# An mLSTM followed by two dense layers: the order of the TensorE program from block 1 on, two steps at a time

## The chip, the cores and the metric

The kernel runs on one core of a Trainium2 chip (trn2). The metric is the device time of one execution in microseconds (us); lower is better. Before the change the median of three runs was 830.93 us (830.81 to 833.44).

## What is computed

```python
# attention: batch 4, heads 8, sequence 768, head size 40, all float32
for t in range(S):
    m_new = np.maximum(f_gate[:, :, t] + m, i_gate[:, :, t])
    f_stab = np.exp(f_gate[:, :, t] + m - m_new)
    i_stab = np.exp(i_gate[:, :, t] - m_new)
    C = f_stab * C + i_stab * outer(v_t, k_t)
    n = f_stab * n + i_stab * k_t
    y[:, :, t] = sigmoid(o_gate_t) * (C @ q_t) / max(abs(n . q_t), 1)
x = y as [3072 tokens, 320]
# first dense layer (320 -> 2048 -> 320)
h = x @ w_in;  g = relu(h) ** 2;                x = g @ w_out
# second dense layer, its own weights
h = x @ w_in2; g = where(h > 0, h, exp(h) - 1); x = g @ w_out2
```

## The kernel before, in words

**Tiles, blocks and steps.** The 3072 tokens are 24 tiles of 128 (tile g is chunk g // 4 of batch g % 4). Three tiles (384 tokens) are a block, 8 blocks make a dense layer, and the two layers are blocks 0 to 7 and 8 to 15. The hidden size 2048 is cut into 16 slices of 128 (`NF`). A **step** is one slice of one block: step t is slice j = t % 16 of block t // 16, 256 steps in all.

**The two products of a step.** TensorE makes the hidden values of a step with `first_product(t)` (line 990, matmuls on line 1000), called F(j) here: 8 matmuls of 128x384 into one of two PSUM banks, `hps[t % 2]`. Values are split in a high and a low part, of which the products that matter are summed. `second_product(t)` (line 1004, matmuls on line 1014), called S(j), adds the step's part to the three accumulators of the block: 9 matmuls of 128x320 into `acc`. S runs `LAG = 3` steps behind F. F(j) waits until the values of step j - 2 have been read from its bank (`relu_ready` in layer one, `g_ready` in layer two); S waits for `glo_ready` of its step.

**Between F and S, layer one.** ScalarE takes relu (line 576), squares it into the high part `ghi` (579) and into `gfull` (580); VectorE subtracts the two to get the low part `glo` (825). ScalarE's relu of step t waits for `glo` of step t - 2, since `relu` and `gfull` have two buffers.

**Between F and S, layer two.** VectorE takes the minimum with zero (857), ScalarE the exponential (618), VectorE the combination (862, `g_ready`), ScalarE the high part (623), GpSimd the low part (456).

**The attention** of tiles 3 to 23 is spread over the steps of blocks 0 to 6 of layer one. `start_of(g)` gives the step s in which a tile starts; `tile_at(t, delay)` finds the tile with s + delay = t. From block 1 on the three tiles of a block start at slices 15 (of the block before), 4 and 9; they are called A, B and C here. On TensorE: `scores` in step s (line 889), `state_added` and `from_state` in step s + 2 (905, 916), `within` in step s + 3 (925). On VectorE: `weigh` in s (659), `gate_recip` in s + 2 (648), `update_state`, `add_inter` and, behind `glo`, `finish` in s + 3 (690 to 707), the transposes of the tile's result in s + 4 (`turned`, 721, 16 instructions), `x_lo` in s + 5 (712), which makes the input of the next block ready (`xt_ready`), and `split_k_lo` of the next tile in its step s - 2 (644). On ScalarE: `exponents` (494), `split_k_hi` in s - 3 (468), `split_q_hi` in s - 2 (473), `x_hi` in s + 5 (509), which waits for the transposes. On GpSimd: `mask` (372) in s - 3, `make_wv` (384) in s - 2, `split_q_lo` in s - 1 (367, two instructions).

**Layer two** has no attention. VectorE transposes the next block's input (721) in the 12 slices of `X2_TURNS`, two instructions behind the minimum and two behind the combination, and makes its low part (`x2_lo`, 733) in slices 5 and 10 behind the combination and in slice 15 ahead of the minimum. It waits each time for `x2_hi` (504) on ScalarE.

**What sets the order.** Each engine runs its own list in program order, written out by hand; semaphores tie them together. TensorE's list before is F(j), the attention of step j, S(j - 3), for each j; at j = 0 the second product comes first and there is none behind. So F(0) and F(1) of a block already stand side by side, and so do the second products of slices 12 and 13. ScalarE's `empty_acc` (526) copies the finished accumulators of a block out in step 2 of the next.

Of the kernel before, what the change touches and what calls it, by code (L numbers as in the profile page):

```python
# [20 lines left out]
NF = FF // P  # L21
T = 3
NT = T * P
BLOCKS = TILES // T
# [36 lines left out]
def tile_at(t, delay):  # L61

    for g in range(T, TILES):
        if start_of(g) + delay == t:
            return g
    return None
# [13 lines left out]
def mlstm_two_dense_layers(nc, gates_ends, gates_inner, qk, q_trios, kvo, w_all, m_dram, out):  # L80
    with ExitStack() as ctx:
# [382 lines left out]
        def _(act):  # L464
# [61 lines left out]
            def empty_acc(block):  # L526
                for u in range(T):
                    i = T * block + u
                    act.wait_ge(s["g_used"], T * (NF * (block + 1) - 1) + u + 1)
                    if block < BLOCKS:  # L530
                        nc.scalar.activation(x2[:, i, :], acc[u][:, 0:DM], ACT.Copy).then_inc(s["acc_free"], 1)
                    else:
                        wait_stage = 16 * (block - BLOCKS)
                        if wait_stage:
                            act.wait_ge(out_done[u], wait_stage)
                        nc.scalar.activation(out_stage[u], acc[u][:, 0:DM], ACT.Copy).then_inc(s["acc_free"], 1)
# [33 lines left out]
            for block in range(2 * BLOCKS):  # L570
                for j in range(NF):
                    t = NF * block + j
                    if block < BLOCKS:
                        act.wait_ge(s["h_ps"], t + 1)
                        wait(act, "glo_ready", t - 1)
                        nc.scalar.activation(relu[t % 2], hps[t % 2][:, 0:NT], ACT.Relu).then_inc(s["relu_ready"], 1)  # L576
                        act.wait_ge(s["relu_ready"], t + 1)
                        wait(act, "g_used", T * (t - GR + 1))
                        nc.scalar.activation(ghi[t % GR][:], relu[t % 2], ACT.Square).then_inc(s["ghi_ready"], 1)  # L579
                        nc.scalar.activation(gfull[t % 2], relu[t % 2], ACT.Square).then_inc(s["g_ready"], 1)  # L580
                        if t + EARLY < NF:
                            split_hi(t + EARLY)
                            split_out_hi(t + EARLY)
                        if FROM_ACT <= t + RING + EARLY - BEHIND < NF:
                            load_w(act, t + RING + EARLY - BEHIND)
                        g = tile_at(t, -5)
                        if g is not None and g >= B:
                            exponents(g, 0)
                        g = tile_at(t, -4)
                        if g is not None and g >= B:  # L590
                            exponents(g, 1)
                        g = tile_at(t, -3)
                        if g is not None and g >= B:
                            split_k_hi(g)
                        g = tile_at(t, -2)
                        if g is not None and g >= B:
                            split_q_hi(g)
                        g = tile_at(t, -1)
                        if g is not None and g >= B:
                            out_gate(g)  # L600
                        if t in FIRST_STATES:
                            first_state(FIRST_STATES[t])
                        g = transposed_at(t)
                        if g is not None:
                            x_hi(g, (g // T) % 2, g % T, A2 if g < 2 * T else x1_turned)
                        if j == LAG - 1 and block > 0:
                            empty_acc(block - 1)
                        if block == BLOCKS - 1:
                            if j >= 1:
                                split_hi(NF + j - 1)  # L610
                            if j >= LAG + 1:
                                split_out_hi(NF + j - LAG - 1)
                            if j in X2_STEPS:
                                w = X2_STEPS.index(j)
                                x_hi(TILES + w, 0, w, (A0, A1, A2)[w])
                    else:
                        act.wait_ge(s["hneg_ready"], t - NF * BLOCKS + 1)
                        nc.scalar.activation(relu[t % 2], relu[t % 2], ACT.Exp).then_inc(s["e_ready"], 1)  # L618
                        if j == LAG - 1:
                            empty_acc(block - 1)  # L620
                        act.wait_ge(s["g_ready"], t + 1)
                        act.wait_ge(s["g_used"], T * (t - GR + 1))
                        nc.scalar.activation(ghi[t % GR][:], gfull[t % 2], ACT.Copy).then_inc(s["ghi_ready"], 1)  # L623
                        if block == BLOCKS and j < LAG + 1:
                            if j == 0:
                                split_hi(2 * NF - 1)
                            split_out_hi(2 * NF - LAG - 1 + j)
                        if block < 2 * BLOCKS - 1 and j in X2_HI_STEPS:
                            w = X2_HI_STEPS.index(j)
                            x2_hi(T * (block + 1 - BLOCKS) + w, (block + 1) % 2, w)  # L630
# [242 lines left out]
        def _(pe):  # L873
            def scores(g):
                if g < B:
                    pe.wait_ge(s[f"qk_in_{g}"], 16)
                    q_h, k_h = q_raw(g), k_raw(g)
                else:
                    pe.wait_ge(s["k_lo"], with_state(g) + 1)
                    q_h, k_h = q3, k3  # L880
                if g >= T:
                    pe.wait_ge(s["den_ready"], g)
                if g == T:
                    pe.wait_ge(s["decay_ready"], 1)
                for u, bank in enumerate(score_banks(g)):
                    if g >= B:
                        pe.wait_ge(s["q_lo"], 2 * with_state(g) + u + 1)
                    for h in range(HH):
                        last = nc.tensor.matmul(bank[:, h * P:(h + 1) * P], k_h[:, u * HH + h, :], q_h[:, u * HH + h, :],  # L889
                                                start=True, stop=True)  # L890
                    last.then_inc(s["s_ps"], 1)

            def state_added(g):
                if chunk_of(g) == CH - 1:
                    return
                pe.wait_ge(s["wv_ready"], g + 1)
                if g == 0:
                    pe.wait_ge(s["a_col_ready"], 2)
                elif g <= T:
                    pe.wait_ge(s["state_ready"], g)  # L900
                else:
                    pe.wait_ge(s["xt_ready"], min(g, 2 * T))
                    pe.wait_ge(s["state_ready"], g)
                for h in range(H):
                    last = nc.tensor.matmul(A2[0:D, h * E:(h + 1) * E], k_of(g)[:, h, :], wv[:, h, :], start=True, stop=True)  # L905
                last.then_inc(s["dc_ps"], 1)
# [111 lines left out]
                if j < NF - 1:  # L1018
                    last.then_inc(s["g_used"], T)

            for block in range(2 * BLOCKS):
                for j in range(NF):
                    t = NF * block + j
                    if j == 0 and block > 0:
                        second_product(t - LAG)
                    first_product(t)
                    if t in FIRST_STATES:
                        state_added(FIRST_STATES[t])
                    g = tile_at(t, 0)
                    if g is not None:  # L1030
                        scores(g)
                    g = tile_at(t, 2)
                    if g is not None:
                        if g > T:
                            state_added(g)
                        from_state(g)
                    g = tile_at(t, 3)
                    if g is not None:
                        within(g)
                    if block == BLOCKS - 1 and j in X2_STEPS:  # L1040
                        w = X2_STEPS.index(j)
                        x2_transposed(w, w)
                    if t >= LAG and j > 0:
                        second_product(t - LAG)
                    g = transposed_at(t)
                    if g is not None and g < 2 * T:
                        x1_transposed(g)
            for t in range(2 * BLOCKS * NF - LAG, 2 * BLOCKS * NF):
                second_product(t)

# [44 lines left out]
```

## Time and profile before

| | |
|---|---|
| median of three runs | 830.93 us |
| the profiled execution, its own time | 832.15 us |
| its span | 830.3 us |
| TensorE matmul busy | 824.3 us, 99% |
| TensorE weight load busy | 813.5 us, 98% |
| VectorE busy | 634.7 us, 76% |
| ScalarE busy | 492.8 us, 59% |
| GpSimd busy | 260.6 us, 31% |
| share of the chain that ended last, by engine | PE 96%, DVE 2%, DMA 1%, ACT 1% |

The span is the time from the first to the last instruction of the program; the execution's own time holds the launch around it. PE is TensorE's matmuls, PEld its weight loads, DVE VectorE, ACT ScalarE, POOL GpSimd, SP SyncE. L1000 is line 1000 of the kernel. The chain that ended last is followed back from the last instruction, at each step to what released it.

### The profile page before, as it was taken

What the parts mean: (1) busy time and instruction counts of PE and PEld (TensorE: products, weight loads), DVE (VectorE), ACT (ScalarE), POOL (GpSimd) and SP (SyncE); (2) the same over time, 40 slices, a digit from 0 to 9 for tenths busy, and PEclk for the clock granted to TensorE, in tenths of its full rate; (3) what the DMA queues carried; (4) which work ended last, traced back from release to release, by engine and by line L of the source; (5) the groups of instructions that cost most, each with busy time, mean ns of one, the idle gap of its engine ahead of it and who ended that gap; (6) DMA issues with size and microseconds to landing.
All of it is one profiled execution on the core that took longest, in us unless ns stands there. A gap on an engine that the chain in (4) does not pass through costs nothing.

```text
span 830.3 us, 15300 instructions
## 1 busy us (share of the span) xinstructions
PE 824.3 (99%) x5451; PEld 813.5 (98%) x5451; DVE 634.7 (76%) x1447; ACT 492.8 (59%) x1088; POOL 260.6 (31%) x270
## 2 busy tenths in 40 slices
PE   9999999999999999999999999999999999999998
PEld 7899999999999999999999999999999999999998
DVE  5798798888897988987966687777868777777642
ACT  4698675776766867678657754444444444444433
POOL 2664222322222222212102353333333333333332
DMA  7785444353653444445132300000000000000000
GB/s 250 241 229 149 136 119 110 109 132 90 160 150 80 140 119 110 109 110 147 46 105 70 106 3 4 27 4 26 2 28 3 28 3 27 4 26 5 2 24 25
DMA packets 29939, 67.64 MB, mean 81 GB/s; under 512 B 9736, under 2 KB 17064, under 8 KB 27304
## 3 DMA queue, kind: packets, MB, share of 16 engines
q1 hardware_dynamic: 29288, 65.23, 27.8%
q10 hardware_dynamic: 576, 1.44, 0.5%
q8 instruction: 43, 0.70, 0.3%
q14 instruction: 32, 0.26, 0.1%
HBM read 60.87 MB, written 4.03 MB: 78 GB/s over the span
## 4 chain that ended last, share of the span: by engine, by line
PE 96%; DVE 2%; DMA 1%; ACT 1%; issue 0%; POOL 0%; DVEq 0%
PE hps L1000 44%; PE acc L1014 41%; PE att L925 5%; PE att L889 2%; PE att L916 2%; PE att L905 2%; DMA wts<-m_rows 1%; ACT wts L494 1%; DVE gate L648 0%; DMA m_rows<-x 0%; DVE wts L659 0%; DMA x<-in_gates_ends 0%; PE att L930 0%; DVE x L704 0%; DVE xtl L712 0%
## 5 line engine op out<-in xcount | busy, mean ns | idle before, releaser
L1000 PE MATMUL hps<-xth,win 128*128 128x384 f32 x1280 | 351.4, 340 | 0.0
L1014 PE MATMUL acc<-wout,ghi 128*128 128x320 f32 x1536 | 345.0, 311 | 0.0
L1000 PE MATMUL hps<-xtl,win 128*128 128x384 f32 x768 | 260.2, 339 | 0.0
L1014 PEld LDWEIGHTS acc<-wout,ghi 128*128 128x128 f32 x1536 | 259.4, 188 | 0.0
L1014 PE MATMUL acc<-wout,glo 128*128 128x320 f32 x768 | 237.4, 309 | 0.0
L1000 PEld LDWEIGHTS hps<-xth,win 128*128 128x128 f32 x1280 | 230.1, 189 | 0.3
L456 POOL TENSOR_TENSOR glo<-hact,ghi 128x384 fp32r<-128x384 f32 x128 | 130.2, 1018 | 215.4 <-ACT ghi L623 215.4
L1000 PEld LDWEIGHTS hps<-xtl,win 128*128 128x128 f32 x768 | 145.0, 189 | 0.0
L1014 PEld LDWEIGHTS acc<-wout,glo 128*128 128x128 f32 x768 | 144.0, 188 | 0.0
L618 ACT ACTIVATE hact<-hact 128x384 f32<-128x384 f32 x128 | 67.4, 526 | 122.3 <-DVE hact L857 122.3
L825 DVE TENSOR_TENSOR glo<-hact,ghi 128x384 fp32r<-128x384 f32 x128 | 75.9, 593 | 66.0 <-ACT hact L580 65.1
L623 ACT ACTIVATE ghi<-hact 128x384 fp32r<-128x384 f32 x128 | 67.3, 526 | 74.6 <-DVE hact L862 74.6
L576 ACT ACTIVATE hact<-hps 128x384 f32<-128x384 f32 x128 | 61.9, 483 | 82.5 <-PE hps L1000 82.5
L857 DVE TENSOR_SCALAR hact<-hps 128x384 f32<-128x384 f32 x128 | 71.1, 556 | 41.7 <-PE hps L1000 39.9
L862 DVE SCALAR_TENSOR_TENSOR hact<-hact,hps 128x384 f32<-128x384 f32 x128 | 71.0, 554 | 28.1 <-ACT hact L618 26.1
L721 DVE STREAM_TRANSPOSE x<-x 32x96 f32<-32x96 f32 (+1 forms) x336 | 84.9, 253 | 7.4
L372 POOL TENSOR_SCALAR_AFFINE_SELECT wts<-wts 128x1024 f32<-128x1024 f32 x24 | 26.3, 1096 | 188.8 <-ACT wts L494 188.6
L721 DVE STREAM_TRANSPOSE x_turned<-x 32x96 f32<-32x96 f32 x288 | 77.6, 269 | 3.6
L367 POOL TENSOR_TENSOR q<-raw,q 40x512 fp32r<-40x512 f32 x40 | 51.9, 1316 | 79.9 <-ACT q L473 79.7
L579 ACT ACTIVATE ghi<-hact 128x384 fp32r<-128x384 f32 x128 | 67.2, 525 | 4.0
L580 ACT ACTIVATE hact<-hact 128x384 f32<-128x384 f32 x128 | 65.0, 508 | 0.0
L494 ACT ACTIVATE wts<-wts,a_col 128x128 f32<-128x128 f32 x192 | 60.4, 387 | 2.1 <-DMA wts<-m_rows 2.1
(142 smaller groups left out, 729.7 us busy)
## 6 DMA issues: line engine op xcount, KB each, us to landing
raw<-in_qk SPq DMA_DIRECT2D x20, 960.0 KB, 7.1
wts<-m_rows SPq DMA_DIRECT2D x24, 512.0 KB, 8.5
kvo<-in_kvo SPq DMA_DIRECT2D x21, 484.0 KB, 7.9
x<-in_w_all SPq DMA_DIRECT2D x12, 352.0 KB, 5.5
wts<-in_w_all SPq DMA_DIRECT2D x12, 352.0 KB, 3.0
q_of_three<-in_q_trios SPq DMA_DIRECT2D x20, 180.0 KB, 2.7
out_x<-hsum SPq DMA_DIRECT2D x16, 160.0 KB, 1.9
x<-in_w_all ACTq DMA_DIRECT2D x4, 352.0 KB, 5.8
```

The source lines that it names most:

```text
L456: nc.gpsimd.tensor_tensor(glo[t % GR][:], gfull[t % 2], f32(ghi[t % GR][:]), ALU.subtract)\
L494: nc.scalar.activation(w[:, h, :], w[:, h, :], ACT.Exp, bias=a_col[:, c, r:r + 1], scale=-1.0).then_inc(s["exp_ready"], 1)
L579: nc.scalar.activation(ghi[t % GR][:], relu[t % 2], ACT.Square).then_inc(s["ghi_ready"], 1)
L580: nc.scalar.activation(gfull[t % 2], relu[t % 2], ACT.Square).then_inc(s["g_ready"], 1)
L618: nc.scalar.activation(relu[t % 2], relu[t % 2], ACT.Exp).then_inc(s["e_ready"], 1)
L623: nc.scalar.activation(ghi[t % GR][:], gfull[t % 2], ACT.Copy).then_inc(s["ghi_ready"], 1)
L721: last = nc.vector.transpose(blocks[q * 32:(q + 1) * 32, 0:n], rows[:, q::4])
L825: nc.vector.tensor_tensor(glo[t % GR][:], gfull[t % 2], f32(ghi[t % GR][:]), ALU.subtract)\
L857: nc.vector.tensor_scalar(relu[t % 2], hps[t % 2][:, 0:NT], 0.0, None, ALU.min).then_inc(s["hneg_ready"], 1)
L862: nc.vector.scalar_tensor_tensor(out=gfull[t % 2], in0=relu[t % 2], scalar=-1.0, in1=hps[t % 2][:, 0:NT], op0=ALU.add, op1=ALU.max).then_i ...
L1000: last = nc.tensor.matmul(hps[t % 2][:, 0:NT], win[:, j, w, :], x[:, kk, :], start=(i == 0), stop=(i == len(parts) - 1))
L1014: last = nc.tensor.matmul(acc[u][:, 0:DM], g[t % GR][:, cols], wout[:, j, w, :], start=(j == 0 and i == 0), stop=(j == NF - 1 and i == 2))
```

## The change

TensorE's program is reordered from block 1 on, and ScalarE's `empty_acc` is put one step earlier to go with it. No instruction is added or taken away. The attention part of a step becomes a function, with its calls in the order that they had. Block 0 keeps its order. From block 1 on TensorE takes slices j and j + 1 together: F(j), F(j + 1), the attention of both, then two second products. With the second product that stands first at j = 0, the list of a block is

S(13) F0 F1 S(14) S(15) | F2 F3 S0 | F4 F5 S1 S2 | F6 F7 S3 S4 | F8 F9 S5 S6 | F10 F11 S7 S8 | F12 F13 S9 S10 | F14 F15 S11 S12

where S(13) to S(15) are of the block before, and the attention of each pair stands behind its two F.

```diff
-                        if j == LAG - 1 and block > 0:
+                        if j == LAG - 2 and block > 0:
                             empty_acc(block - 1)
...
-                        if j == LAG - 1:
-                            empty_acc(block - 1)
                         act.wait_ge(s["g_ready"], t + 1)
                         act.wait_ge(s["g_used"], T * (t - GR + 1))
                         nc.scalar.activation(ghi[t % GR][:], gfull[t % 2], ACT.Copy).then_inc(s["ghi_ready"], 1)
+                        if j == LAG - 2:
+                            empty_acc(block - 1)
...
+            def attention(t):
+                block, j = divmod(t, NF)
+                if t in FIRST_STATES:
+                    state_added(FIRST_STATES[t])
+                g = tile_at(t, 0)
+                if g is not None:
+                    scores(g)
+                g = tile_at(t, 2)
+                if g is not None:
+                    if g > T:
+                        state_added(g)
+                    from_state(g)
+                g = tile_at(t, 3)
+                if g is not None:
+                    within(g)
+                if block == BLOCKS - 1 and j in X2_STEPS:
+                    w = X2_STEPS.index(j)
+                    x2_transposed(w, w)
+
+            for t in range(NF):
+                first_product(t)
+                attention(t)
+                if t >= LAG:
+                    second_product(t - LAG)
+                g = transposed_at(t)
+                if g is not None:
+                    x1_transposed(g)
+            for block in range(1, 2 * BLOCKS):
+                for j in range(0, NF, 2):
                     t = NF * block + j
-                    if j == 0 and block > 0:
+                    if j == 0:
                         second_product(t - LAG)
                     first_product(t)
...
-                    if t >= LAG and j > 0:
-                        second_product(t - LAG)
...
+                    first_product(t + 1)
+                    attention(t)
+                    attention(t + 1)
+                    if j != 2:
+                        second_product(t - LAG + (j == 0))
+                    second_product(t - LAG + 1 + (j == 0))
```

## Rows read from the trace of the kernel before

**Rows 1.** The page's line of busy time, share of the span and instructions by engine.

```profile
PE 824.3 (99%) x5451; PEld 813.5 (98%) x5451; DVE 634.7 (76%) x1447; ACT 492.8 (59%) x1088; POOL 260.6 (31%) x270
```

**Rows 2.** Waits of TensorE: who for whom, us in total, times, longest.

```profile
PE att L889 <- issue: 0.5, 2, 0.3
```

**Rows 3.** Timeline, TensorE, layer two: start us, us, engine, line, operation, tiles, count.

```profile
588.91 0.51 PE L1000 MATMUL hps<-xth,win 128*128 128x384 f32 x2
...
590.32 0.45 PE L1014 MATMUL acc<-wout,ghi 128*128 128x320 f32 x2
...
591.63 0.51 PE L1000 MATMUL hps<-xth,win 128*128 128x384 f32 x2
...
603.96 0.45 PE L1014 MATMUL acc<-wout,ghi 128*128 128x320 f32 x2
...
606.59 0.51 PE L1000 MATMUL hps<-xth,win 128*128 128x384 f32 x2
...
609.39 0.45 PE L1014 MATMUL acc<-wout,ghi 128*128 128x320 f32 x2
```

**Rows 4.** Timeline, VectorE and ScalarE, slices 10, 11 and 12 of a layer-two block.

```profile
590.52 0.56 DVE L857 TENSOR_SCALAR hact<-hps 128x384 f32<-128x384 f32 x1 [0.50 <-PE hps L1000]
...
593.23 1.06 DVE L733 TENSOR_TENSOR xtl<-x,xth 128x384 fp32r<-128x384 f32 x1 [1.01 <-ACT xth L504]
...
598.70 0.56 DVE L857 TENSOR_SCALAR hact<-hps 128x384 f32<-128x384 f32 x1
...
600.44 0.49 DVE L721 STREAM_TRANSPOSE x<-x 32x64 f32<-32x64 f32 x2
```

**Rows 5.** Timeline, VectorE and TensorE: a wait for `den_ready` (L704) ends at scores.

```profile
92.17 0.49 DVE L704 TENSOR_TENSOR x<-att,rden 128x320 f32<-128x320 f32 x1
...
92.76 0.41 PE L889 MATMUL att<-q,k 120*128 120x128 f32 x2 [0.25 <-issue]
```

**Rows 6.** Timeline, TensorE, end of a layer-one block: within, S9, and F0 of the next.

```profile
252.86 1.87 PE L925 MATMUL att<-kvo,wts 128*128 128x41 f32 x16
254.56 0.53 PE L1014 MATMUL acc<-wout,ghi 128*128 128x320 f32 x2
...
266.37 0.51 PE L1000 MATMUL hps<-xth,win 128*128 128x384 f32 x2
```

**Rows 7.** Timeline, VectorE, the same stretch: tile C from finish to x_lo.

```profile
255.03 0.50 DVE L690 TENSOR_TENSOR att<-hsum,att 128x328 f32<-128x328 f32 x1
...
256.99 0.20 DVE L707 COPY x<-x 128x64 f32<-128x64 f32 x1
257.22 1.22 DVE L644 TENSOR_TENSOR k<-raw,k 40x1024 fp32r<-40x1024 f32 x1
...
259.06 0.56 DVE L825 TENSOR_TENSOR glo<-hact,ghi 128x384 fp32r<-128x384 f32 x1 [0.62 <-ACT hact L580]
259.54 4.51 DVE L721 STREAM_TRANSPOSE x_turned<-x 32x96 f32<-32x96 f32 x16
...
264.65 0.56 DVE L712 TENSOR_TENSOR xtl<-x_turned,xth 128x384 fp32r<-128x384 f32 x1
```

**Rows 8.** Timeline, ScalarE and GpSimd, the same stretch.

```profile
254.42 1.04 ACT L468 ACTIVATE k<-raw 120x1024 fp32r<-120x1024 f32 x1
...
257.57 0.49 ACT L576 ACTIVATE hact<-hps 128x384 f32<-128x384 f32 x1 [2.10 <-PE hps L1000]
...
258.94 1.04 ACT L473 ACTIVATE q<-raw 120x1024 fp32r<-120x1024 f32 x1
```

**Rows 9.** Timeline, GpSimd: `split_q_lo` in block 0, and at that block end.

```profile
86.18 2.88 POOL L367 TENSOR_TENSOR q<-raw,q 40x512 fp32r<-40x512 f32 x2 [0.90 <-ACT q L473]
...
260.06 2.55 POOL L367 TENSOR_TENSOR q<-raw,q 40x512 fp32r<-40x512 f32 x2 [6.28 <-ACT q L473]
```

**Rows 10.** Timeline, VectorE: `glo` beside the first of these, a copy beside another.

```profile
86.39 1.54 DVE L825 TENSOR_TENSOR glo<-hact,ghi 128x384 fp32r<-128x384 f32 x1
...
352.10 1.16 DVE L707 COPY x<-x 128x64 f32<-128x64 f32 x1
```

More of the change, by code:

```diff
@@ L1019, in second_product @@
                     last.then_inc(s["g_used"], T)
-            for block in range(2 * BLOCKS):
-                for j in range(NF):
+            def attention(t):
[16 more added lines that the diff above has]
+                    x2_transposed(w, w)
@@ L1026, in _ @@
                     first_product(t)
[L1027 to L1039, printed above, removed]
@@ L1040, in _ @@
-                    if block == BLOCKS - 1 and j in X2_STEPS:
-                        w = X2_STEPS.index(j)
-                        x2_transposed(w, w)
-                    if t >= LAG and j > 0:
-                        second_product(t - LAG)
-                    g = transposed_at(t)
-                    if g is not None and g < 2 * T:
-                        x1_transposed(g)
+                    first_product(t + 1)
[3 more added lines that the diff above has]
+                        second_product(t - LAG + (j == 0))
```

## The prediction

> **What bounds the kernel now.** I read the page's line of busy times first: TensorE's matmuls are busy 824.3 of 830.3 us [rows 1]. Then the waits of TensorE: behind the start-up there is nearly nothing, two waits of 0.5 us together at the scores, both in block 0, whose order stays [rows 2]. So no wait is there to be removed. A change of order can shorten the matmul stream itself, where two neighbours cost less than others, and it can bring waits where an answer of another engine is now due earlier. The timelines give both. All times below are starts of matmuls, since recorded ends overlap.
>
> **The stream itself.** In layer two F takes 1.41 us up to the next S, and S 1.31 us up to the next F; two steps are 5.44. Two S side by side take 2.63, two F side by side 2.80, together 5.43 [rows 3]. Read to a hundredth the gain is 0.01 per pair; the rounding allows 0 to 0.03, and I take 0.02. Each block had one such pair and gets eight, so 7 x 15 x 0.02 = 2.1 us less. In the six pairs where tile B's `from_state` and `within` meet, one change between attention and products falls away; I take 0.03 us each (0 to 0.1). **Together -2.3 us (0 to -3.7).**
>
> **Layer one, end of a block.** Tile C: `within` (slice 12) now runs behind F13. F0 of the next block needs C's `x_lo`. I set the start of S9, the first product behind `within`, to 0. Before, F0 came at 266.37 - 254.56 = 11.81 [rows 6]. Now F13 is no longer between the two: F0 is due at 11.81 - 1.42 = 10.39. From the end of an awaited VectorE operation to the matmul is 0.10 us (92.66 to 92.76) [rows 5], so `x_lo` has to end by 10.29.
> - VectorE: `within` ends 0.17 behind S9's start (252.86 + 1.87) [rows 6], `finish` starts at 0.21. Its copy (L707) starts 1.96 later, so 2.17 to 2.37; then the k part (L644), 1.22, to 3.62; `glo` of 13 at 3.65, which before had to wait 0.62 for ScalarE and now doesn't, as F13 is earlier; from the start of `glo` to the end of `x_lo` 265.21 - 259.06 = 6.15 [rows 7]. End 9.80: undisturbed, 0.49 us of slack are left where the trace of before has 1.16.
> - GpSimd: `split_q_lo` of the next tile A follows ScalarE. F12 starts at -(1.70 + 2.80) = -4.50 (`within` takes 254.56 - 252.86 [rows 6]); relu 1.61 later, as in layer two the minimum (590.52 - 588.91 [rows 3, 4]), at -2.89; the k copy (L468) 1.37 later, 1.04 long, to -0.48; relu of 13; the q copy (L473) 1.37 later, 1.04 long, to 1.93 [rows 8]. GpSimd starts 0.08 later, at 2.0, and runs 2.55, to 4.55 [rows 9]. Before it ran wholly beside the transposes, which it doesn't hurt (4.51 us beside it [rows 7]).
> - So the copy at 2.17 and the k part at 2.4 now meet GpSimd. A copy of 0.20 us [rows 7] took 1.16 beside it, and `glo`, 0.56 alone, took 1.54 when it started 0.21 behind it, ending 0.46 behind the first of the two GpSimd instructions [rows 9, 10]. The copy waits for the first (3.3), the k part for the second: it is the same kind of operation as `glo`, a difference of two SBUF tensors, but no row shows it started well inside one. It ends at 4.55 + 1.1 = 5.65, `x_lo` at 5.7 + 6.15 = 11.8, F0 1.5 us late. Lower bound: the k part isn't held, `glo` is, until 4.5: 4.5 + 6.15 = 10.65, 0.4 late. Upper: the copy is held by both: 1.7 late. I take 1.5, since the nearest row is `glo`'s.
> - Five block ends have a tile A behind the C (tiles 8, 11, 14, 17, 20): **+7.5 us (1.8 to 8.5).**
>
> The Trainium skill (SBUF — State Buffer, "Who interferes with whom") says that a VectorE instruction with two SBUF inputs contends with a GpSimd instruction that reads SBUF, as an exclusive lock: who starts first has it for its whole instruction. By that rule the k part is held too, which is the 1.5; the trace agrees with it at `glo`, 1.54 against 0.56 us. It speaks against this change, and a count of TensorE's work alone would not show it.
>
> **Layer two.** Here VectorE's work comes in bursts: F(j) and F(j + 1) end 1.4 us apart, and VectorE needs 2.2 us for a step with transposes (598.70 to 600.93, of it 1.71 to `g_ready`) [rows 4].
> - F5 waits for `g_ready` of 3. F2 starts at 0; minimum at 1.61; next minimum at 3.87; ready at 5.58, matmul at 5.68. F5 is due at 2.80 + 1.31 + 1.41 = 5.52, since this pair has one S only. 0.16 late.
> - F13 waits for `g_ready` of 11, which stands behind `x2_lo` of slice 10. From F10's start `x2_lo` ends 5.38 later (594.29) [rows 3, 4], since it follows ScalarE and GpSimd, which keep their distance; the minimum of 11 starts at 5.3, ready at 7.0, matmul at 7.1. F13 is due at 2.80 + 2.63 + 1.41 = 6.84. 0.26 late.
> - Blocks 8 to 14 have both: 7 x 0.42 = 2.9, and 0.3 in block 8, where ScalarE splits the last weights too. **+3.2 us (0, if what VectorE does is picked up earlier, to 5).**
>
> **What costs nothing.** S gets its `glo` with more room than before (four or more S and F between, 6.9 us at least, against 1.7 us from F's end to `g_ready` and, as an estimate, as much again for `ghi` and `glo`). `empty_acc` is done 1.1 us ahead of S(0). F7 of layer one, which needs the relu behind tile A's transposes, keeps 0.7 us; if a GpSimd operation held up VectorE there for 1.2, it would cost 0.5 a block. DMAs wait for `within` or `from_state` of tiles two or three back, and the earliest is needed five steps later.
>
> **Sum.** Span 830.3 - 2.3 + 7.5 + 3.2 = 838.7. The profiled execution was 832.15 with that span, so 840.6 by its own time; the median of the runs lies 1.22 lower: **839.3 us**.
>
> **Rivals.**
> - *The k part isn't held* (0.22): 5 x 0.4 = 2.0 in place of 7.5: 830.9 - 2.3 + 2.0 + 3.2 = 833.8. For it: it works on 40 partitions and not on 128 [rows 7], and `glo` [rows 10] got its turn between the two GpSimd instructions. Against it: that turn is then the copy's.
> - *The scores of tile C wait as well* (0.12): tile B's `glo` of 7 starts inside `split_q_lo` of C. Held by its first half, `finish` ends 0.35 us ahead of the scores of C; held by both halves, 1.3 later: 0.9 us in six blocks, 844.7.
> - *Only layer two waits* (0.14): GpSimd starts after 3.6, as ScalarE is later than I count, and the 0.49 holds: 830.9 - 2.3 + 3.2 = 831.8.
> - *Faster* (0.07): the stream alone is left. That needs the 0.49 of slack at F0 to hold (`split_q_lo` not before 3.6, or not in the way) and `g_ready` of 11 by 6.74 instead of 7.0. Then 830.9 - 2.3 = 828.6. Against it: the rows leave no room for 0.26 us in a chain that repeats to 0.02.
>
> The forecast has 0.45. A change under 0.3% (2.5 us, 828.4 to 833.4) can't be told from none; 828.6 is just inside, so part of that case counts as same, which I round up for what the stream may give beyond 2.3. Slower: 0.45 + 0.12 + two thirds of 0.22 = 0.71. Faster 0.06, same 0.23. The range goes from 831.0 (under the layer-two case) to 843.0; below lies the faster case, above most of the case with the scores.
>
> **What would show it.** Waits of TensorE at line 1000 on VectorE's L712, five times about 1.5 us, at the ends of blocks 1 to 5; on L862, 14 times, 0.16 and 0.26 us; beside `split_q_lo` a copy (L707) of over 1 us and a k part (L644) of over 2 us at five places. Between waits a pair of layer two takes 5.43. Wrong it would be if L644 stays at 1.22, or if `split_q_lo` starts behind it.

## The result

The kernel after takes 841.92 us (median of four runs, 840.52 to 842.68), the kernel before 831.70 in the same comparison: 1.012 times as long, 95% interval 1.0103 to 1.0138. The forecast was 839.3 us, with a range of 831.0 to 843.0 and a chance of 0.71 that it is slower. It is slower and inside the range; the loss is 10.2 us where 8.4 were forecast. Executions of one kernel fall into two groups some 1 us apart, by the mean granted clock that they report (the kernel before, timed beside e8, e10 and e11: mean 831.5 us over the 16 that report about 0.98, 832.6 over the 7 that report 1.00).

### The profile page after: what moved, and what is told of

Read it like the earlier page. It is cut to its first block, busy times and chain, and to the rows that moved or that the text cites. A ratio compares the mean times of both kernels' runs of the same rounds, so it can differ in the third digit from the quotient of the medians.

```text
span 840.9 us, 15300 instructions
## 1 busy us (share of the span) xinstructions
PE 825.9 (98%) x5451; PEld 808.1 (96%) x5451; DVE 638.1 (76%) x1447; ACT 489.9 (58%) x1088; POOL 261.1 (31%) x270
## 4 chain that ended last, share of the span: by engine, by line
PE 88%; DVE 8%; issue 2%; DMA 1%; ACT 0%; SPq 0%; DVEq 0%
PE hps L1000 41%; PE acc L1014 36%; PE att L925 5%; DVE x_turned L721 2%; PE att L916 2%; PE att L889 2%; PE att L905 2%; DVE k L644 1%; DMA raw<-in_qk 1%; DVE glo L825 1%; DVE gate L648 0%; DVE x L704 0%; DVE x L721 0%; DVE xtl L712 0%; PE acc L889 0%
## 5 line engine op out<-in xcount | busy, mean ns | idle before, releaser
L825 DVE TENSOR_TENSOR glo<-hact,ghi 128x384 fp32r<-128x384 f32 x128 | 79.9, 624 | 54.2 <-ACT hact L580 53.3
L367 POOL TENSOR_TENSOR q<-raw,q 40x512 fp32r<-40x512 f32 x40 | 53.8, 1362 | 67.3 <-ACT q L473 67.2
```

The lines of the kernel that those rows point to most:

```text
L825: nc.vector.tensor_tensor(glo[t % GR][:], gfull[t % 2], f32(ghi[t % GR][:]), ALU.subtract)\
```

## The profile after

The page's line of busy times of the kernel after; before it was [rows 1].

```profile
PE 825.9 (98%) x5451; PEld 808.1 (96%) x5451; DVE 638.1 (76%) x1447; ACT 489.9 (58%) x1088; POOL 261.1 (31%) x270
```

The span is 840.9 us, 10.6 more, but matmuls are busy only 1.6 us more. The rest is idle time between them. These are four rows of the waits of TensorE in the kernel after (line waited at, releaser, us in total, times, longest); before, `xtl` L712 stood at no matmul of line 1000.

```profile
PE hps L1000 <- DVE xtl L712: 5.2, 5, 1.1
PE att L889 <- issue: 1.7, 3, 1.2
PE acc L889 <- DMA raw<-in_qk: 1.5, 1, 1.5
PE hps L1000 <- DVE hact L862: 0.2, 1, 0.2
```

The first row is of the change. The second and third lie ahead of block 1, where the order is unchanged. The longest wait of the second row, 1.2 us, ends at the scores at 58.4 us, in block 0, and makes most of the 0.9 us by which this execution takes longer than the one before from F0 of block 0 to F0 of block 1. The wait for the DMA is at 14.7 us, in the start-up; F0 of block 0 comes 0.4 us earlier than before all the same. Both waits differ from run to run and are no part of the change.

The fourth row is nearly all that this view has of layer two, where 15 first products come 0.1 to 0.3 us late. The recorded end of a matmul lies behind the start of the next, so a short wait leaves little or no idle time in the record. For layer two the starts of the matmuls have to be read.

**By block.** The start of F0 of each block in the timelines of before and after gives every block's length; block 15 is taken up to the last second product. The table shows the difference to the kernel before, in us:

| blocks | after - before | what it is |
|---|---|---|
| 1, 2, 3, 4 | +1.20, +1.27, +1.26, +1.27 | F0 of the next block late |
| 5 | +1.66 | the same, and tile C's `from_state` waits |
| 6 | +0.31 | tile C's `from_state` waits |
| 7 | -0.14 | no wait |
| 8 | +0.93 | F5, F9 and F13 late |
| 9 to 14 | +0.39 to +0.41 each | F5 and F13 late |
| 15 | -0.14 | no wait |

Blocks 1 to 7 sum to 6.8 us, 8 to 15 to 3.2. Of the 10.6 us of the span, 0.4 are ahead of block 1 and 0.2 behind the last second product.

**The end of a layer-one block**, the kernel after. These three timelines are of VectorE, GpSimd and TensorE (with one of its weight loads) in block 3; [rows 6, 7, 9] are the same place before.

```profile
259.03 0.51 DVE L690 TENSOR_TENSOR att<-hsum,att 128x328 f32<-128x328 f32 x1 [1.04 <-PE att L925]
...
261.00 1.06 DVE L707 COPY x<-x 128x64 f32<-128x64 f32 x1
262.09 2.24 DVE L644 TENSOR_TENSOR k<-raw,k 40x1024 fp32r<-40x1024 f32 x1
264.36 0.56 DVE L825 TENSOR_TENSOR glo<-hact,ghi 128x384 fp32r<-128x384 f32 x1
264.84 4.50 DVE L721 STREAM_TRANSPOSE x_turned<-x 32x96 f32<-32x96 f32 x16
269.37 0.56 DVE L825 TENSOR_TENSOR glo<-hact,ghi 128x384 fp32r<-128x384 f32 x1
269.93 0.56 DVE L712 TENSOR_TENSOR xtl<-x_turned,xth 128x384 fp32r<-128x384 f32 x1
```

```profile
260.71 2.53 POOL L367 TENSOR_TENSOR q<-raw,q 40x512 fp32r<-40x512 f32 x2 [4.00 <-ACT q L473]
```

```profile
257.12 1.87 PE L925 MATMUL att<-kvo,wts 128*128 128x41 f32 x16
258.82 0.39 PE L1014 MATMUL acc<-wout,ghi 128*128 128x320 f32 x1
...
264.38 0.97 PEld L889 LDWEIGHTS att<-q,k 120*128 120x128 f32 x8 [0.20 <-DVE k L644]
...
270.54 0.44 PE L1000 MATMUL hps<-xth,win 128*128 128x384 f32 x1 [1.05 <-DVE xtl L712]
```

What to look at is how the two engines alternate. GpSimd starts at 260.71. VectorE's copy, 0.20 us alone, starts at 261.00 and ends at 262.06, when the first of the two GpSimd instructions is over (half of 2.53 us). The k part starts behind it, beside the second, and ends at 264.33, 1.09 us behind GpSimd's end (263.24): it takes 2.24 instead of 1.22 us. The transposes start 1.9 us later than they would (0.86 and 1.02 added), `x_lo` ends at 270.49, and F0 starts 0.05 us behind that, 1.2 us late. The held k part costs a little at a second place: the scores of tile A wait for it (the weight load at 264.38) and take 0.94 instead of 0.84 us up to the next product.

**Slices 10 to 13 of a layer-two block**, the kernel after: first VectorE, then TensorE with its weight loads; before, [rows 3, 4].

```profile
599.28 0.56 DVE L857 TENSOR_SCALAR hact<-hps 128x384 f32<-128x384 f32 x1 [0.95 <-PE hps L1000]
...
601.99 1.06 DVE L733 TENSOR_TENSOR xtl<-x,xth 128x384 fp32r<-128x384 f32 x1 [1.01 <-ACT xth L504]
602.97 0.55 DVE L857 TENSOR_SCALAR hact<-hps 128x384 f32<-128x384 f32 x1
603.55 0.55 DVE L721 STREAM_TRANSPOSE x<-x 32x96 f32<-32x96 f32 x2
604.11 0.55 DVE L862 SCALAR_TENSOR_TENSOR hact<-hact,hps 128x384 f32<-128x384 f32 x1
```

```profile
604.34 0.34 PE L1000 MATMUL hps<-xtl,win 128*128 128x384 f32 x1
604.71 0.30 PEld L1000 LDWEIGHTS hps<-xth,win 128*128 128x128 f32 x2 [0.36 <-DVE hact L862]
604.72 0.62 PE L1000 MATMUL hps<-xth,win 128*128 128x384 f32 x2
605.00 0.19 PEld L1000 LDWEIGHTS hps<-xtl,win 128*128 128x128 f32 x1
605.17 0.34 PE L1000 MATMUL hps<-xtl,win 128*128 128x384 f32 x1
```

The minimum of 11 (602.97) stands behind `x2_lo` (601.99, 1.06 us). F13's first matmul follows the last of F12 by 0.38 us (604.34 to 604.72) where 0.17 is usual: it is 0.21 late. The second is late as well: two matmuls take 605.17 - 604.72 = 0.45 instead of some 0.35. The weight loads of both start only at 604.71; the rows show none made ahead during the wait.

## The experiments

Each run was timed beside the kernel before. `L1` and `L2` are the differences in length of blocks 1 to 7 and 8 to 15 to the kernel before, taken from the profiled execution of each, in us; the ratio is that of all its runs to those of the kernel before. Of e12 there is one execution only, so it has no interval and is used for its profile.

| run | L1 | L2 | ratio (95%) |
|---|---|---|---|
| after | +6.8 | +3.2 | 1.0120 (1.0103 to 1.0138) |
| e1_layer_two_only | 0.0 | +3.1 | 1.0040 (1.0028 to 1.0053) |
| e2_layer_one_only | +6.9 | 0.0 | 1.0063 (1.0043 to 1.0084) |
| e3_no_q_low_of_a | -0.4 | +3.1 | 1.0025 (1.0014 to 1.0036) |
| e4_12_and_13_apart | +3.7 | +3.2 | 1.0087 (1.0069 to 1.0105) |
| e5_low_part_at_11 | +6.8 | +0.8 | 1.0097 (1.0076 to 1.0119) |
| e6_no_turns_at_3 | +6.9 | +3.0 | 1.0112 (1.0087 to 1.0138) |
| e7_k_part_first | +0.6 | +3.2 | 1.0049 (1.0033 to 1.0064) |
| e9_zeros_at_10 | +6.8 | +0.8 | 1.0098 (1.0079 to 1.0116) |
| e8_no_turns_at_2 | +6.8 | +2.5 | 1.0116 (1.0102 to 1.0131) |
| e10_three_mended | +0.6 | +0.1 | 1.0008 (0.9998 to 1.0019) |
| e11_pairs_where_free | -0.6 | -1.0 | 0.9981 (0.9971 to 0.9991) |
| e12_longer_zeros | +6.8 | +0.8 | 1.008 (one execution) |

**One layer alone.** The loop over pairs runs the old order inside, where a condition says so:

```diff
                 for j in range(0, NF, 2):
+                    if block < BLOCKS:          # e1; e2: block >= BLOCKS
+                        for i in (j, j + 1):
+                            t = NF * block + i
+                            if i == 0:
+                                second_product(t - LAG)
+                            first_product(t)
+                            attention(t)
+                            if i > 0:
+                                second_product(t - LAG)
+                        continue
```

> Pairs only from block 8 on, layer one and its emptying of the accumulators as before the change. Theory (each layer pays by itself): layer two costs +0.4 us in each of blocks 8 to 14 (F5 0.2 late, F13 0.3 late, less 0.14 for the stream) and some 0.5 more in block 8: +3.2 us against the kernel before, 1.004; no wait of TensorE at line 1000 on L712. Rival (the loss of layer two is carried over from a late layer one, or from the start-up): +0 to 1 us.

> Pairs only in blocks 1 to 7, layer two as before the change. Theory: five waits of 1.2 us at F0 of blocks 2 to 6, in all +6.5 to +7 us against the kernel before, 1.008; blocks 9 to 15 start as far behind as block 8. Rival (layer two catches up or loses with it): under +5 or over +9.

The blocks in the old order are as long as before to 0.01 us each, in either run. The losses are local and add: 3.1 and 6.9 us, together 10.0.

**Is it GpSimd, or only the burst (VectorE's work on the tile coming behind two first products at once)?**

```diff
-                            split_q_lo(g, 0)
-                            split_q_lo(g, 1)
+                            if g % T == 0 and g > 2 * T:
+                                pool.wait_ge(s["q_hi"], with_state(g) + 1)
+                                pool.sem_inc(s["q_lo"], 2)
+                            else:
+                                split_q_lo(g, 0)
+                                split_q_lo(g, 1)
```

> The kernel after, but GpSimd leaves out split_q_lo of the tiles A from 9 on (five tiles, 10 instructions): their q keeps only its rounded value. Theory (GpSimd holds VectorE's copy and k part by turns): copy back to 0.20 us, L644 to 1.22, F0's waits of 1.2 us gone in blocks 2 to 6, 6.0 us faster than the kernel after, +4 against before (1.005). Rival (the burst alone: finish stands behind F13 and that is already too late): the copy and L644 shorter, but F0 still 0.5 to 1.2 us late, under 3 us faster than after.

VectorE at the same place in this run (its lines are four further down):

```profile
258.89 0.20 DVE L711 COPY x<-x 128x64 f32<-128x64 f32 x1
259.12 1.22 DVE L648 TENSOR_TENSOR k<-raw,k 40x1024 fp32r<-40x1024 f32 x1
260.37 0.56 DVE L829 TENSOR_TENSOR glo<-hact,ghi 128x384 fp32r<-128x384 f32 x1
```

Copy and k part are back to 0.20 and 1.22, `x_lo` ends 0.59 us ahead of F0 at the five block ends, and no F0 waits for it. Blocks 1 to 4 are now 0.16 us shorter than before. Layer one gains 7.2 us on the kernel after, more than the 6.0 expected, since each late F0 also cost 0.1 at the matmul behind it, and the scores of A, which no longer wait for the k part, take 0.84 us again instead of 0.94. The burst alone is no loss; the meeting is.

**Taking the pair apart where tile C ends.**

```diff
+                    if block < BLOCKS - 1 and j == 12:   # then as in e1
```

> The kernel after, but in layer one the slices 12 and 13 are taken one at a time as before (F12, within, S9, F13, S10); the GpSimd work stays. Theory: within of tile C is 1.4 us earlier against the rest, finish and the k part are over before GpSimd starts, F0 waits no more: 6 us faster than the kernel after, less 0.1 for the stream, +4 against before (1.005). Rival (any of the pairs before it makes VectorE late): F0 still late by 0.5 us or more in each block.

F0 waits no more, its `x_lo` is 1.96 us ahead, but only 3.1 of the 6 us come. The waits of TensorE in this run:

```profile
PE att L889 <- POOL q L367: 2.6, 5, 0.5
```

And at one of the five places:

```profile
264.05 0.64 PE L889 MATMUL att<-q,k 120*128 120x128 f32 x4
265.20 0.66 PE L889 MATMUL att<-q,k 120*128 120x128 f32 x4 [0.51 <-POOL q L367]
```

The scores of A now wait for `split_q_lo` itself: with F13 later and F14 and F15 still a pair, they come 1.3 us earlier in relation to it than in the kernel before. Neither theory had that; it is the same GpSimd work, asked for too early instead of met.

**The k part in VectorE's idle time.**

```diff
-                        if g is not None and g >= B:
+                        if g is not None and g >= B and not (block > 0 and j == 13):
                             split_k_lo(g)
...
+                        g = tile_at(t, -3)
+                        if g is not None and block > 0 and j == 12:
+                            split_k_lo(g)
                         g = tile_at(t, 3)
                         if g is not None:
                             finish(g)
```

> The kernel after, but in slice 12 of layer one VectorE makes the k part of the next tile A ahead of finish instead of behind it, in the 1.0 us in which it waits for within. Theory (not the amount of work, but that it meets GpSimd's two instructions in turn): L644 back to 1.22, finish 0.6 us later, its copy held by the first GpSimd instruction and glo by the second, transposes some 1.2 us earlier than in the kernel after, x_lo 0.1 us ahead of F0: the five waits of 1.2 us shrink to 0 to 0.15 each, 5.5 to 6 us faster than the kernel after. Rival (whatever comes last is held, and the delay stays about the sum of the GpSimd work): F0 still 0.6 us late or more.

VectorE and GpSimd in this run:

```profile
255.08 1.22 DVE L644 TENSOR_TENSOR k<-raw,k 40x1024 fp32r<-40x1024 f32 x1 [0.39 <-ACT k L468]
...
258.30 0.46 DVE L707 COPY x<-x 128x64 f32<-128x64 f32 x1
258.69 1.68 DVE L825 TENSOR_TENSOR glo<-hact,ghi 128x384 fp32r<-128x384 f32 x1
```

```profile
257.42 2.53 POOL L367 TENSOR_TENSOR q<-raw,q 40x512 fp32r<-40x512 f32 x2 [4.00 <-ACT q L473]
```

GpSimd holds VectorE here too, the copy by 0.26 and `glo` by 1.12, but the 1.22 of the k part are over by then. Blocks 1 to 4 are as long as before to 0.06 us; F0 is still some 0.1 late, which eats the stream's gain. With the same amount of work and the same GpSimd instructions, 6.3 us of the 6.8 come back.

**Layer two: what stands in front of slice 11's minimum.**

```diff
-X2_LO_STEPS = (5, 10, 15)
+X2_LO_STEPS = (5, 11, 15)
```

> The kernel after with VectorE's x2_lo of slice 10 moved behind slice 11 (X2_LO_STEPS 5, 11, 15). Theory (x2_lo stands in the way of slice 11's minimum, since F11 now ends 1.4 us behind F10): g_ready of 11 comes 1.9 us earlier, F13's wait of 0.3 us is gone in blocks 8 to 14, F5's stays: 2.2 us faster than the kernel after (0.9974 of it). Rival (VectorE has simply more than it can do in a burst of two slices): the wait moves to F15 or F0, no gain.

All of F13's wait is gone and nothing came in its place: blocks 9 to 14 are 0.05 to 0.09 us longer than before instead of 0.40. But the run changes two things. `x2_lo` now starts 0.1 us ahead of GpSimd's subtraction, and is no longer long itself; GpSimd's is, 1.33 instead of 1.02 us:

```profile
601.45 0.56 DVE L733 TENSOR_TENSOR xtl<-x,xth 128x384 fp32r<-128x384 f32 x1
601.55 1.33 POOL L456 TENSOR_TENSOR glo<-hact,ghi 128x384 fp32r<-128x384 f32 x1 [0.96 <-ACT ghi L621]
```

The next run leaves `x2_lo` in its place and takes away what GpSimd reads beside it:

```diff
-                        nc.gpsimd.tensor_tensor(glo[t % GR][:], gfull[t % 2], f32(ghi[t % GR][:]), ALU.subtract)\
-                            .then_inc(s["glo_ready"], 1)
+                        if j == 10:
+                            nc.gpsimd.memset(f32(glo[t % GR][:]), 0.0).then_inc(s["glo_ready"], 1)
+                        else:                            # as before
```

> The kernel after, but in slice 10 of the blocks of layer two GpSimd writes zeros as the low part of g instead of the difference, so it reads nothing from SBUF there. Theory (x2_lo is held by GpSimd's reads): x2_lo takes 0.56 instead of 1.06 us in slice 10, g_ready of 11 comes 0.5 us earlier, F13's wait is gone: 2.2 us faster than the kernel after. Rival (x2_lo is held by any GpSimd operation, or takes 1.06 by itself): it stays at 1.06, or ends with the zeros' end, and F13 waits as before.

`x2_lo` takes 0.56 instead of 1.06 and F13 waits no more, as much gained as in the run before. So F13's wait needs both, `x2_lo` in front of the minimum and its length. But the zeros are written in 0.42 us and are over 0.03 us behind `x2_lo`'s start, so this run doesn't tell GpSimd's reads from any operation of it. A last one puts a longer write in front:

```diff
+                            nc.gpsimd.memset(raw[:, 0, :], 0.0)
                             nc.gpsimd.memset(f32(glo[t % GR][:]), 0.0).then_inc(s["glo_ready"], 1)
```

> As the run with zeros in slice 10, but GpSimd first writes zeros over 120x1024 of a buffer that layer two doesn't use, and then the 128x384 of the low part, so that x2_lo starts well inside a GpSimd operation that only writes. Theory (what holds x2_lo is GpSimd's reading): x2_lo takes 0.56 us beside the long write, and F13's wait stays away. Rival (any GpSimd operation holds it): it ends some 0.4 us behind the end of the long write, 1.1 us or more after its start, and F13 is as late as in the kernel after or later.

```profile
600.23 0.56 DVE L737 TENSOR_TENSOR xtl<-x,xth 128x384 fp32r<-128x384 f32 x1 [1.00 <-ACT xth L508]
```

```profile
599.84 0.96 POOL L457 MEMSET raw<- 120x1024 f32 x1 [2.12 <-ACT ghi L625]
600.74 0.42 POOL L458 MEMSET glo<- 128x384 f32 x1
```

VectorE's subtraction starts 0.39 us into a GpSimd write and runs through it in 0.56, in all seven blocks. Beside GpSimd's subtraction, 0.37 us into it, it took 1.06. These writes don't hold it; what held it was an operation that reads.

**Layer two: F5.**

```diff
-X2_TURNS = (0, 1, 2, 3, 4, 6, 7, 8, 9, 11, 12, 13)
+X2_TURNS = (0, 1, 2, 4, 5, 6, 7, 8, 9, 11, 12, 13)    # e6
+X2_TURNS = (0, 1, 3, 4, 5, 6, 7, 8, 9, 11, 12, 13)    # e8
```

> The kernel after with the transposes of slice 3 in layer two moved to slice 5. Theory: the pair of slices 2 and 3 has one second product behind it, so F5 is due 1.3 us earlier than elsewhere and is the only F that a slice with transposes makes late; without them F5's wait of 0.23 us is gone in blocks 8 to 14, 1.6 us faster than the kernel after. Rival: it comes back at F7, whose slice has the transposes now and x2_lo behind them: no gain.

The theory missed: blocks 9 to 14 are as long as in the kernel after. VectorE in slices 2 and 3 of this run:

```profile
576.93 0.55 DVE L862 SCALAR_TENSOR_TENSOR hact<-hact,hps 128x384 f32<-128x384 f32 x1
577.51 0.49 DVE L721 STREAM_TRANSPOSE x<-x 32x64 f32<-32x64 f32 x2
578.01 0.56 DVE L857 TENSOR_SCALAR hact<-hps 128x384 f32<-128x384 f32 x1
579.16 0.55 DVE L862 SCALAR_TENSOR_TENSOR hact<-hact,hps 128x384 f32<-128x384 f32 x1 [0.59 <-ACT hact L618]
```

The combination of 3 still comes 1.15 us behind its minimum: without transposes between, VectorE waits the 0.59 us for the exponential. Those transposes were free. What delays the minimum (578.01) are the two behind the combination of slice 2.

> The kernel after with the transposes of slice 2 of layer two moved to slice 5 (slice 3 keeps its own). In the run with slice 3 free of them F5 was as late as before, because the transposes behind the minimum fall into the wait for ScalarE's exponential. New theory: only those behind slice 2's combination stand in the way, since they hold up the minimum of slice 3 by 0.5 us; g_ready of 3 then comes 0.5 us after 4.56 instead of 5.56 us behind F2's start, F5's wait of 0.23 us is gone in blocks 8 to 14, 1.6 us faster than the kernel after. Rival (the minimum of 3 is late for the next thing in the chain anyway): F5's run of 16 matmuls stays at 3.03 us.

With those moved, F4 and F5 together take 2.80 us instead of 3.00 to 3.03, and blocks 9 to 14 are 0.19 longer than before instead of 0.40. Block 8, where VectorE splits the last weights in slice 3, is the worse for it (1.5 instead of 0.9), which the expectation had not weighed.

**Everything mended, and the version that is left.**

> The kernel after with the three mended together: k part first in slice 12 of layer one, x2_lo behind slice 11, no transposes in slice 2 of layer two. Theory (the three waits are apart and add): blocks 2 to 5 of layer one as long as before the change, blocks 5 and 6 0.35 us longer each (from_state of C waits there), blocks 9 to 14 0.14 us shorter each than before, block 8 0.3 to 0.9 longer: -0.3 to +0.7 us against the kernel before (1.000). Rival (mending one brings up another): blocks 9 to 14 longer than before by 0.1 us or more.

The three add: blocks 9 to 14 are 0.13 to 0.15 us shorter than before each. What remains are 0.39 and 0.31 us in blocks 5 and 6 and 1.1 in block 8. The time can't be told from that of the kernel before.

```diff
+def paired(block, j):
+    return block > BLOCKS or block == BLOCKS - 1 or 1 <= block <= 4 and j < 12
```

> Pairs only where no run showed a wait: in blocks 1 to 4 the slices 0 to 11, all of block 7, and blocks 9 to 15 with x2_lo behind slice 11 and no transposes in slice 2; the rest in the order before the change. Theory (two F side by side cost 0.028 us less, two S 0.008 more): 0.14 us less in each of blocks 7 and 9 to 15, 0.1 less in blocks 1 to 4, 1.5 us faster than the kernel before (0.998), at the edge of what the measurement tells. Rival (the stream's gain is not real or is eaten by waits): 1.000 or above.

0.9981 (0.9971 to 0.9991): the stream's gain is real, 1.6 us by the blocks of the profile, and with these waits avoided it is faster than both kernels. The median of twelve runs is 830.99 us against 831.67. Their difference is less than 1.6, since the kernel before has more of the executions that report a clock of 0.98; within either group of executions e11 is 1.8 and 1.5 us faster by the means.

## Why the prediction came out as it did

- **The bound and the sign: right.** TensorE's stream was closed before [rows 1, 2], so the change had little to win and several margins to lose. Shown by e11 (what there was to win) and by e1 and e2.
- **The stream, -2.3 us: right.** A block without waits is 0.14 us shorter (7 x 0.02). The 0.03 for tile B was not there: side by side `from_state` and `within` take 2.48 us between starts, apart 2.39, which eats the change saved. As much came at slices 8 and 9, where tile C's scores are (0.045 us less for that pair, not 0.02), so the sum is right partly by luck.
- **The end of a layer-one block, +7.5: right in each step, and 7.2 by what e3 takes away.** The copy fell into the first GpSimd instruction (0.29 us behind its start, forecast 0.17), the k part into the second, and L644 ended 1.09 behind GpSimd (forecast 1.1). Against the 1.5 forecast for a block end, F0 was only 1.2 us late: `x_lo` ended 0.1 earlier than counted, the matmul followed it by 0.05 us and not 0.10, and F0 was due 0.14 later, because the scores in front of it waited for the k part. But that wait is a loss of its own, as is 0.1 behind F0 with the second weight load, and with them a block end costs 1.4. The sum of the prediction had neither. e3 shows the cause by taking it away, e7 by moving what it met.
- **Layer two, F5 and F13: right in place and chain, the sizes off by two terms.** The minimum of 3 starts 3.85 us behind F2 (forecast 3.87), that of 11 starts 5.31 behind F10 (forecast 5.3). The first matmuls were 0.09 and 0.21 us late, forecast 0.16 and 0.26, since they start 0.05 behind the end of the combination and not 0.10. The second matmul adds 0.11 each time, which the sum doesn't have. Together 0.20 to 0.23 and some 0.33. e8 removes the first; e5 and e9 each remove the second. The prediction named `x2_lo`'s place but not that half its length is the same GpSimd hold.
- **The first experiment on F5 was built on a wrong reading.** The prediction's 3.87 has the transposes behind slice 2's combination in it. Reading it as "a slice with transposes is late" led to e6, which moved the wrong two.
- **Layer two as a whole, +3.2: too small by 1.1.** Of this, 0.1 are in each of blocks 9 to 14, and block 8, where F9 is late too, cost 0.5 more than the others, not 0.3. Net of the stream layer two cost 3.2, forecast 2.1.
- **A wait that the sum put at nothing without a reason: `from_state` of tile C in blocks 5 and 6.** These tiles belong to the last chunk, which has no `state_added`, so `from_state` follows F11 at once, 0.8 us earlier than elsewhere. In block 5 of the kernel after, VectorE and TensorE:

```profile
365.13 1.28 DVE L659 TENSOR_TENSOR wts<-wts,att 128x512 f32<-128x512 f32 x2
...
365.50 0.34 PE L1000 MATMUL hps<-xtl,win 128*128 128x384 f32 x1
...
365.95 0.46 PE L916 MATMUL att<-state_diag,q_of_three 120*128 120x126 f32 x2
```

  `from_state` waits for the first half of `weigh`, which ends some 0.7 us after 365.13. It starts 0.45 us behind F11's last matmul, where 0.18 is usual, and with the matmuls behind it some 0.4 us are lost in each of the two blocks. In e11, where these blocks keep the old order, they are as long as before. The prediction worked through a tile with all its parts and not through the last chunk, which has fewer.
- **The scores of tile C, a rival at 0.12: did not happen.** Tile B's `glo` was held by the first half only, as the likelier reading of [rows 10] had it; the scores of C start 0.8 us behind the end of L704 in blocks 1 to 4, where 0.1 would mean a wait.
- **How near the total came is in part luck.** By blocks the loss is 10.0 us where the terms give 8.4. `from_state` (0.8) and layer two (1.1) were missing, and the block ends were counted 0.3 too high.

The Trainium skill (SBUF — State Buffer, "Who interferes with whom") had said that a VectorE instruction with two SBUF inputs is held by a GpSimd instruction that reads SBUF, and not by one that only writes. Both halves hold here: 2.24 against 1.22 us at L644, and 0.56 beside a write where it was 1.06 beside a read. That a copy is held too stands there for the modes that use two ports; L707's 1.06 against 0.20 agrees, though no run here shows in which mode it ran.

## What to carry to other kernels

When one engine has no idle time left, a new order for it is a change of due times for all others: for each wait, redo the time at which the answer is due and the time at which it is ready, with the work that the answering engine has in front, for the first, the typical and the last block separately. Look for what two engines will now do at the same time, not only for what waits for what: here a 1.2 us subtraction that had stood alone met GpSimd, and where it was put into idle time the loss was gone. And before moving work out of a chain, see whether it lies in a wait of that chain; if it does, moving it brings nothing.

## What the runs showed of the hardware that was not expected

- Two instructions of GpSimd right behind each other don't keep VectorE out: it gets its turn between them. The copy ended at the first one's end (262.06), and where `glo` got the turn, GpSimd's second instruction was longer by some 0.3 us (2.88 for the two [rows 9] against 2.53). When VectorE's subtraction starts first, it is GpSimd's that takes longer, and by no more than 0.3 us (e5: 1.33 against 1.02).
- After a wait, TensorE loses a further 0.1 us at the second matmul: gaps of 0.38 and 0.28 us at F13, where 0.17 is usual. The wait explains the first; at the second, the rows show its weight load not made ahead.
- The granted clock of the view is no guide to the start-up. It reads 0.62 in the first 40 us of the kernel after and 1.00 in those of the kernel before, where TensorE is busy for 37.4 of the 40. But in the kernel before, too, matmuls of 384 columns follow each other by 0.32 us, the pace of the lower level (1.2 GHz), until 40.6 us, and by 0.17 from then on (2.4 GHz):

```profile
38.71 0.52 PE L1000 MATMUL hps<-xtl,win 128*128 128x384 f32 x1
39.03 0.84 PE L1000 MATMUL hps<-xth,win 128*128 128x384 f32 x2
...
40.63 0.34 PE L1000 MATMUL hps<-xtl,win 128*128 128x384 f32 x1
40.81 0.34 PE L1000 MATMUL hps<-xth,win 128*128 128x384 f32 x1
```

  In the kernel after the pace changes at 39.5 us, in e1, whose view reads 1.00 as well, at about 41. From there on all read 1.00. Block 1 starts only at 97 us, so the loss is not the clock's. What the executions that report 0.98 have is a short stretch at the upper level early on: at 6 us the kernel after makes 16 matmuls of L889 in 2.05 us, the kernel before 13 in 3.14. That this is why they are some 1 us shorter is likely and not tested.
